# Sparse attention and two feed-forward stages: the values as the stationary operand, the probabilities divided by their sums on GpSimd

## The chip, the core and the metric

The program runs on one core of a Trainium2 chip. What is measured is the device time of one execution in microseconds, from the first to the last instruction. TensorE does the matmuls, VectorE the search and elementwise work, ScalarE activations and copies out of PSUM, GpSimd (POOL in the profile) elementwise work in SBUF; SyncE issues the transfers. The engines run side by side, each its own instructions in order, and wait for each other by semaphores.

## What is computed

Attention over 4 batches, 8 heads, 576 tokens and 64 dimensions a head, in which each query keeps its 32 best keys, and then two feed-forward stages over all 2304 tokens:

```python
scores = scale * np.matmul(q, k.transpose(0, 1, 3, 2))
kth = np.partition(scores, -top_k, axis=-1)[..., -top_k:-top_k + 1]   # top_k = 32
scores = np.where(scores >= kth, scores, -1000000000.0)
attn = np.exp(scores - np.max(scores, axis=-1, keepdims=True))
attn = attn / (np.sum(attn, axis=-1, keepdims=True) + 1e-09)
x = np.matmul(attn, v)                      # heads side by side: 2304 x 512
h = x @ w_in                                # 512 x 2048
x = (h / (1.0 + np.exp(-1.702 * h))) @ w_out
out = (((x @ w1) * (x @ w2)) @ w3) @ w_out2
```

## The kernel before

**Tiles and slots.** The 2304 tokens are eight chunks of 288 queries, two to a batch. A chunk has 18 tiles (`CT`), two groups of nine (`GT`), a group for four heads. Tile `r == 0` of a group is the left tile: the last 32 queries of each of the four heads, 128 rows. The others are 128 queries of one head; heads go in order, `j` being the half of the head's 256 queries. All tiles are in one sequence of 144, and a slot is one tile's turn. Each engine goes through the slots and in each does steps of several tiles, older ones further on: `slot.next(-3)` is the tile three behind.

**A tile's way.** TensorE makes scores two slots ahead (L560); ScalarE copies them to SBUF (L769, a ring of six rows). VectorE searches: four times the eight largest (L979, L987, L993, L999), three times replacing them (L984, L990, L996); the first half in the tile's own slot, the rest in the next. GpSimd scales the 32nd value to a threshold (`scale_threshold`, L1241) at the end of that next slot. In slot +2 ScalarE makes a penalty (L780), GpSimd subtracts it (L1227), ScalarE takes the exponential with its row sum (L789). In slot +3 GpSimd adds 1e-9 to the sum (`add_eps`, L1250), VectorE inverts it (`invert`, L1007), and TensorE transposes the row in five pieces (L573, L574). ScalarE copies them to `probs_T` (L798, L799) and TensorE multiplies, `probs_T` stationary and the values moving (L588): ten instructions in the profile for five matmuls. ScalarE copies the 64 columns out, scaled by the inverse sum (`copy_output`, L817; four pieces of all four heads' product for a left tile, L814). When both heads of a pair are there, TensorE transposes 128x128 of x in slot +4 (`transpose_x`, L603), and in slot +5 ScalarE makes its high half-precision part (`high_xt`, L831) and VectorE the low one (`low_xt`, L1028); for a left tile each in two instructions.

**Feed-forward.** The chunk before the current one, or the one before that, runs through the first feed-forward stage in the same slots: 32 units of twelve fp16 matmuls of 288 columns (L632), two in most slots, one in slots 3, 7, 12 and 16, the first from slot 5. Units 0 to 15 go through ScalarE (tanh L853, copy L856), VectorE (gate L1014), ScalarE (g_high L865) and GpSimd (g_low L1256).

**Preparation.** GpSimd splits the next group's queries into two parts (L1182): per group eight instructions of 256 columns and two of 128, and, when the next group belongs to a new batch, four of 576 for its keys. They lie in slots 1 to 5 of a group's nine. Keys come with even chunks, so the splits with keys stand in slots 1 to 5 of even chunks (for their second group) and in slots 10 to 14 of odd ones (for the first group of the next).

**Order on each engine, per slot.** It is written out by hand. TensorE: transpose_probs(-3), scores(+2), first unit, weigh_values(-3), second unit, transpose_x(-4). ScalarE: high_xt(-5), penalise(-2), second unit's copies, copy_probs(-3), copy_scores(+2), exponentials(-2), high gate, first unit's copies, copy_output(-3), preparation, high gate. VectorE: search of the new and the old tile in turn, gates between, invert(-3) and low_xt(-5) after the old tile's last replacement. GpSimd:

```python
add_eps(slot.next(-3))
subtract_penalty(slot.next(-2))
for c, u in second_unit(slot.next(-2)):
    low_gate(c, u)
negate_max(slot)
prepare(slot)
for c, u in first_unit(slot.next(-1)):
    low_gate(c, u)
scale_threshold(slot.next(-1))
```

**The end.** The second stage begins when all tiles and units are done, at some 975 us, and is matmuls alone.

## Time and profile before

| | us |
|---|---|
| three runs, median | 1276.18 |
| lowest, highest | 1272.49, 1278.28 |
| profiled execution, span | 1276.3 |
| busy: TensorE (weight loads) | 1179.1 (989.6) |
| busy: VectorE | 939.7 |
| busy: ScalarE | 788.3 |
| busy: GpSimd | 544.5 |

The profiled execution has no other time than its span; it equals the median. Busy times are unions: the instructions of one engine overlap at their ends. "L1028 waited for L831" means that the engine was idle before its instruction of line 1028 until one of line 831 released it.

### The profile page before, as it was taken

What the parts mean: (1) busy time and instruction counts of PE and PEld (TensorE: products, weight loads), DVE (VectorE), ACT (ScalarE), POOL (GpSimd) and SP (SyncE); (2) the same over time, 40 slices, a digit from 0 to 9 for tenths busy, and PEclk for the clock granted to TensorE, in tenths of its full rate; (3) what the DMA queues carried; (4) which work ended last, traced back from release to release, by engine and by line L of the source; (5) the groups of instructions that cost most, each with busy time, mean ns of one, the idle gap of its engine ahead of it and who ended that gap; (6) DMA issues with size and microseconds to landing.
All of it is one profiled execution on the core that took longest, in us unless ns stands there. A gap on an engine that the chain in (4) does not pass through costs nothing.

```text
span 1276.3 us, 25043 instructions
## 1 busy us (share of the span) xinstructions
PE 1179.1 (92%) x7798; PEld 989.6 (78%) x7798; DVE 939.7 (74%) x1974; ACT 788.3 (62%) x1806; POOL 544.5 (43%) x905
## 2 busy tenths in 40 slices
PE   2699987799999989999989999999989999999999
PEld 2466565687788877878868787887768999999998
DVE  4999999998999998999999899999442311302302
ACT  3655688867977977886886788797473222222211
POOL 4634445846755675674575666555230000000000
PEclk9799999899999989999999999999999999999999
DMA  9924142311001120000202100000151011011000
GB/s 283 361 60 158 58 128 86 99 35 48 2 26 45 42 65 29 25 11 24 62 22 62 44 11 25 11 7 1 37 206 44 9 41 49 8 41 49 0 25 25
DMA packets 29868, 75.40 MB, mean 59 GB/s; under 512 B 2480, under 2 KB 14256, under 8 KB 27824
## 3 DMA queue, kind: packets, MB, share of 16 engines
q1 hardware_dynamic: 29744, 73.93, 18.6%
q8 instruction: 55, 0.90, 0.3%
q14 instruction: 69, 0.57, 0.1%
HBM read 62.39 MB, written 11.53 MB: 58 GB/s over the span
## 4 chain that ended last, share of the span: by engine, by line
PE 56%; DVE 15%; issue 14%; ACT 6%; POOL 6%; DMA 1%; POOLq 0%; SPq 0%; ACTq 0%; DVEq 0%
PE ff_ps L632 32%; PE values_ps L588 9%; PE scores_ps L632 5%; PE scores_ps L560 4%; PE values_ps L632 3%; PE probs_T_ps L573 2%; DVE search L996 2%; DVE search L990 2%; POOL g_low L1256 2%; DVE top L987 2%; DVE peaks L1032 2%; DVE top L979 2%; DVE search L984 1%; ACT penalty L780 1%; ACT probs_T L798 1%
## 5 line engine op out<-in xcount | busy, mean ns | idle before, releaser
L1227 POOL TENSOR_TENSOR scores<-scores,penalty 128x576 f32<-128x576 f32 x144 | 203.2, 1411 | 196.2 <-ACT penalty L780 196.1
L588 PE MATMUL values_ps<-v_rows,probs_T 128*128 128x64 f32 (+3 forms) x1440 | 226.5, 295 | 53.9 <-ACT probs_T L799 46.3
L588 PEld LDWEIGHTS values_ps<-v_rows,probs_T 128*128 128x128 f32 (+1 forms) x1440 | 194.9, 193 | 100.9 <-ACT probs_T L799 66.0
L1160 DVE TENSOR_TENSOR ab_T<-a_sb,ff_ps 128x384 f32<-128x384 f32 x48 | 26.6, 554 | 211.1 <-PE ff_ps L632 211.1
L632 PE MATMUL ff_ps<-g_high,w_out_high 128*128 128x288 f16 x512 | 149.6, 292 | 2.7 <-DVE w_out_low L1019 1.6
L632 PE MATMUL ff_ps<-x_T_high,w_in_high 128*128 128x288 f16 x512 | 149.1, 291 | 2.9 <-ACT gate L856 2.8
L632 PE MATMUL ff_ps<-g_high,w_out_low 128*128 128x288 f16 x512 | 148.7, 291 | 0.0
L632 PE MATMUL ff_ps<-g_low,w_out_high 128*128 128x288 f16 x512 | 148.7, 290 | 0.0
L632 PE MATMUL ff_ps<-x_T_high,w_in_low 128*128 128x288 f16 x512 | 147.9, 289 | 0.0
L632 PE MATMUL ff_ps<-x_T_low,w_in_high 128*128 128x288 f16 x512 | 147.9, 289 | 0.0
L780 ACT ACTIVATE penalty<-scores,threshold_scaled 128x576 f32<-128x576 f32 x144 | 111.0, 771 | 35.6 <-POOL threshold_scaled L1241 35.1
L789 ACT ACTIVATE scores<-scores,neg_max 128x576 f32<-128x576 f32 x144 | 111.8, 776 | 32.1 <-POOL scores L1227 32.1
L1256 POOL TENSOR_TENSOR g_low<-gate,g_high 128x288 f16<-128x288 f32 x128 | 99.9, 782 | 72.4 <-ACT g_high L865 72.4
L632 PE MATMUL ff_ps<-x_high,w_high 128*128 128x384 f32 x384 | 128.4, 334 | 0.8 <-issue 0.8
L632 PE MATMUL ff_ps<-x_high,w_low 128*128 128x384 f32 x384 | 128.3, 334 | 0.0
L632 PE MATMUL ff_ps<-x_low,w_high 128*128 128x384 f32 x384 | 128.3, 334 | 0.0
L979 DVE MAX8 top<-scores 128x8 f32<-128x576 f32 x144 | 107.8, 749 | 5.8 <-ACT scores L769 3.7
L769 ACT ACTIVATE scores<-scores_ps 128x576 f32<-128x576 f32 x144 | 92.4, 641 | 27.0 <-PE scores_ps L560 26.9
L987 DVE MAX8 top<-search 128x8 f32<-128x576 f32 x144 | 107.5, 747 | 0.5
L999 DVE MAX8 top<-search 128x8 f32<-128x576 f32 x144 | 106.7, 741 | 0.0
L993 DVE MAX8 top<-search 128x8 f32<-128x576 f32 x144 | 106.6, 740 | 0.0
L990 DVE MATCH_REPLACE8 search<-top,search 128x576 f32<-128x576 f32 x144 | 106.6, 740 | 0.0
(116 smaller groups left out, 2777.1 us busy)
## 6 DMA issues: line engine op xcount, KB each, us to landing
q_stage<-q_T SPq DMA_DIRECT2D x32, 288.0 KB, 4.3
k_stage<-k_T SPq DMA_DIRECT2D x16, 576.0 KB, 8.4
x_scratch<-x_out SPq DMA_DIRECT2D x32, 144.0 KB, 1.7
x_T<-x_scratch SPq DMA_DIRECT2D x6, 768.0 KB, 4.8
out<-y_out SPq DMA_DIRECT2D x18, 256.0 KB, 2.0
v_rows<-v_rows_in SPq DMA_DIRECT2D x8, 512.0 KB, 3.6
w_T<-w_T_in SPq DMA_DIRECT2D x1, 4096.0 KB, 26.9
whole_weight<-w_in SPq DMA_DIRECT2D x2, 2048.0 KB, 11.1
```

What stands on the lines that cost most here:

```text
L588: last = nc.tensor.matmul(xp[:, 0:n], pt[0:rows, j * P:(j + 1) * P], vn[0:rows, j, first:first + n], start=j == 0, stop=j == KB)
L632: last = nc.tensor.matmul(out, stationary[i], moving[j], start=first and n == 0, stop=last_one and n == 2)
L769: act.activation(sc[:, t.ring(RING), :].rearrange("p (a b) -> p a b", a=2), ps[:, :, 0:HALF], ACT.Copy).then_inc(s_copied, 1)
L780: act.activation(pen[:, :], sc[:, t.ring(RING), :], ACT.Relu, bias=thr[:, r:r + 1], scale=-PENALTY).then_inc(pen_done, 1)
L789: act.activation(sc[:, t.ring(RING), :], sc[:, t.ring(RING), :], ACT.Exp, bias=negm[:, r:r + 1], scale=SCALE, accum_out=total[:, r:r + 1]) ...
L979: nc.vector.max(tops[:, 0:8], row).then_inc(search_a, 1)
L987: nc.vector.max(tops[:, 8:16], rest).then_inc(search_a, 1)
L990: nc.vector.match_replace(rest, tops[:, 8:16], rest, FLOOR).then_inc(search_a, 1)
L993: nc.vector.max(tops[:, 16:24], rest).then_inc(search_b, 1)
L999: nc.vector.max(tops[:, 24:32], rest).then_inc(search_b, 1)
L1227: pool.tensor_tensor(row, row, pen[:, :], ALU.subtract).then_inc(masked_done, 1)
L1256: pool.tensor_tensor(gt[1][:, u, :], gf[:, u % FF_RING, :], gt[0][:, u, :], ALU.subtract).then_inc(g_low, 1)
```

## The change

The values become the stationary operand (128 keys by one head's 64 dimensions) and the transposed probabilities move (128 queries). The product is then x already transposed, 64 rows by 128 queries, and two heads fill one PSUM tile, the even one in rows 0 to 63 and the odd one in rows 64 to 127. The order of tiles within a group becomes two heads in turn for one half of the queries, so that a pair is complete with every second tile (`ends_group`), and the matmuls of both tiles are issued together, alternating between the heads; a left tile makes its two pairs at once with 32 moving columns for each head. `transpose_x`, `copy_output`, `x_rows` and `x_left` go. Since rows of queries are now columns, the division by the row sum moves ahead of the transposes: `normalise` on GpSimd multiplies the 128x576 row by the inverse in place, in slot +3, and TensorE transposes, copies and weighs in slot +4. The last piece of the row is transposed as its last 128 columns, and `v_rows` holds zeros for the 64 keys that this counts twice. `probs_T` gets two rows, `x_T_ps` two banks; ScalarE copies all 640 columns in one instruction.

```diff
-        self.h, self.j = self.g * HG + (self.r - 1) // 2, (self.r - 1) % 2
+        self.h = self.g * HG + (self.r - 1) // 4 * 2 + (self.r - 1) % 2
+        self.j = (self.r - 1) // 2 % 2
...
+    def ends_group(self):
+        return self.r % 2 == 0
...
             def transpose_probs(t):
-                pe.wait_ge(exp_done, t.count(1))
+                pe.wait_ge(norm_done, t.count(1))
                 wait(pe, pt_copied, t.count())
                 row = sc[:, t.ring(RING), :]
-                for j in range(KB):
-                    nc.tensor.transpose(ptp[:, j * P:(j + 1) * P], row[:, j * P:(j + 1) * P], ident[:, :])
-                nc.tensor.transpose(pte[0:KR, 0:P], row[:, KB * P:S], ident[:, :]).then_inc(transposed, 1)
+                for j in range(KB + 1):
+                    last = nc.tensor.transpose(ptp[:, j * P:(j + 1) * P], row[:, min(j * P, S - P):min((j + 1) * P, S)],
+                                               ident[:, :])
+                last.then_inc(transposed, 1)

             def weigh_values(t):
-                pe.wait_ge(pt_copied, t.count(1))
-                wait(pe, o_copied, t.count())
-                first, n = (t.g * HG * D, HG * D) if t.left else (t.h * D, D)
-                for j in range(KB + 1):
-                    rows = KR if j == KB else P
-                    last = nc.tensor.matmul(xp[:, 0:n], pt[0:rows, j * P:(j + 1) * P],
-                                            vn[0:rows, j, first:first + n], start=j == 0, stop=j == KB)
+                wait(pe, xt_low, t.group_count(-2))
+                wait_alone(pe, pt_copied, t.count(1), passed_pe)
+                out = xq[t.group() % 2]
+                if t.left:
+                    members = [[(t, 2 * pair + odd, slice((2 * pair + odd) * LEFT, (2 * pair + odd + 1) * LEFT),
+                                 slice(pair * LEFT, (pair + 1) * LEFT)) for odd in range(2)] for pair in range(2)]
+                else:
+                    members = [[(t.next(odd - 1), t.next(odd - 1).h % HG, slice(0, P), slice(0, P))
+                                for odd in range(2)]]
+                for pair in members:
+                    for j in range(KB + 1):
+                        for odd, (tile, head, queries, cols) in enumerate(pair):
+                            first = (t.g * HG + head) * D
+                            last = nc.tensor.matmul(
+                                out[odd * D:(odd + 1) * D, cols], vn[:, j, first:first + D],
+                                pt[:, tile.ring(2), j * P + queries.start:j * P + queries.stop],
+                                start=j == 0, stop=j == KB)
                 last.then_inc(av_done, 1)
...
-                    transpose_probs(slot.next(-3))
+                    transpose_probs(slot.next(-4))
...
-                    weigh_values(slot.next(-3))
+                    weigh_values(slot.next(-4))
...
-                    transpose_x(slot.next(-4))
...
             def copy_probs(t):
-                wait(act, av_done, t.count())
-                act.activation(pt[:, 0:KB * P], ptp[:, :], ACT.Copy)
-                act.activation(pt[0:KR, KB * P:(KB + 1) * P], pte[0:KR, 0:P], ACT.Copy
-                               ).then_inc(pt_copied, 1)
+                wait(act, av_done, t.next(-2).group_count())
+                act.activation(pt[:, t.ring(2), :], ptp[:, 0:PADDED], ACT.Copy).then_inc(pt_copied, 1)
...
             def high_xt(t):
-                act.wait_ge(xt_made, t.xt_count(1))
+                act.wait_ge(av_done, t.group_count())
-                for rows, dst, src in xt_parts(t, xt[0]):
-                    last = act.activation(dst, src, ACT.Copy, scale=scale[rows, 0:1])
-                last.then_inc(xt_high, 1)
+                act.activation(xt_place(t, xt[0]), xt_source(t), ACT.Copy, scale=scale[:, 0:1]).then_inc(xt_high, 1)
...
-                    copy_probs(slot.next(-3))
+                    copy_probs(slot.next(-4))
...
-                    copy_output(slot.next(-3))
...
             def low_xt(t):
-                for (rows, dst, src), (_, high, _) in zip(xt_parts(t, xt[1]), xt_parts(t, xt[0])):
-                    last = nc.vector.scalar_tensor_tensor(dst, src, scale[rows, 0:1], high, ALU.mult, ALU.subtract)
-                last.then_inc(xt_low, 1)
+                nc.vector.scalar_tensor_tensor(xt_place(t, xt[1]), xt_source(t), scale[:, 0:1], xt_place(t, xt[0]),
+                                               ALU.mult, ALU.subtract).then_inc(xt_low, 1)
...
+            def normalise(t):
+                wait_alone(pool, recip_done, t.count(1), passed_pool)
+                r = t.ring(4)
+                row = sc[:, t.ring(RING), :]
+                pool.tensor_scalar(row, row, rinv[:, r:r + 1], 1.0, ALU.mult, ALU.mult).then_inc(norm_done, 1)
...
                     for c, u in first_unit(slot.next(-1)):
                         low_gate(c, u)
+                    normalise(slot.next(-3))
                     scale_threshold(slot.next(-1))

-            pool.memset(xl[:, :, :], 0.0).then_inc(ones_set, 1)
+            pool.memset(vn[0:P - KR, KB, :], 0.0).then_inc(zeros_set, 1)
```

## Rows read from the trace of the kernel before

**Rows 1.** Table of stretches: us; busy (instructions) PE, PEld, DVE, ACT, POOL; clock, DMA, GB/s.

```profile
600.00:700.00 100.00, 91.91 (x693) 76.77 (x692) 91.98 (x208) 78.58 (x192) 62.34 (x102) 0.98 0.19 48
1000.00:1100.00 100.00, 100.00 (x534) 94.30 (x533) 20.35 (x35) 22.65 (x40) 0.00 (x0) 1.00 0.09 32
```

**Rows 2.** Waits, 300 to 900 us: who waited for whom, us in total, times, longest.

```profile
POOL scores L1227 <- ACT penalty L780: 140.9, 102, 2.9
...
ACT x_T_high L831 <- PE x_T_ps L603: 22.1, 22, 2.3
...
DVE x_T_low L1028 <- ACT x_T_high L831: 14.9, 17, 1.6
...
DVE inverse_total L1007 <- POOL total_eps L1250: 5.5, 7, 1.1
```

**Rows 3.** The gate on DVE: groups of 300 to 900 and 885 to 1000 us, one instruction.

```profile
L1014 DVE SCALAR_TENSOR_TENSOR gate<-tanh,gate 128x288 f32<-128x288 f32 x96 | 57.9, 603 | 2.1 <-ACT gate L856 2.1
...
L1014 DVE SCALAR_TENSOR_TENSOR gate<-tanh,gate 128x288 f32<-128x288 f32 x17 | 7.3, 453 | 9.4 <-ACT gate L856 9.4
...
658.64 1.16 DVE L1014 SCALAR_TENSOR_TENSOR gate<-tanh,gate 128x288 f32<-128x288 f32 x1
```

**Rows 4.** Table of stretches again: chunks 4 and 5, slots 1-5, 10-14, then slot 17.

```profile
487.70:517.90 30.20, 28.69 (x209) 23.74 (x208) 25.96 (x60) 23.78 (x52) 19.60 (x32) 0.94 0.11 34
541.50:572.20 30.70, 27.66 (x205) 22.19 (x204) 30.43 (x70) 28.19 (x74) 23.46 (x40) 1.00 0.01 2
592.50:620.40 27.90, 27.54 (x211) 22.82 (x210) 25.79 (x61) 21.53 (x50) 15.59 (x30) 1.00 0.05 17
645.60:679.20 33.60, 27.58 (x205) 22.14 (x203) 31.68 (x69) 30.21 (x74) 28.05 (x42) 1.00 0.06 19
...
680.00:700.00 20.00, 20.00 (x152) 17.44 (x151) 18.33 (x43) 11.69 (x27) 8.47 (x18) 0.93 0.41 98
```

**Rows 5.** DVE's waits in 487 to 512, 592 to 615 and 645 to 680 us.

```profile
DVE inverse_total L1007 <- POOL total_eps L1250: 1.4, 2, 0.9
...
DVE x_T_low L1028 <- ACT x_T_high L831: 2.1, 2, 1.1
...
DVE inverse_total L1007 <- POOL total_eps L1250: 1.1, 1, 1.1
```

**Rows 6.** Groups by line on POOL, whole span, shapes apart.

```profile
L1227 POOL TENSOR_TENSOR scores<-scores,penalty 128x576 f32<-128x576 f32 x144 | 203.2, 1411 | 196.2 <-ACT penalty L780 196.1
...
L1182 POOL TENSOR_TENSOR q_high_low<-q_stage,q_high_low 128x256 fp32r<-128x256 f32 x64 | 45.6, 732 | 4.0 <-ACT q_high_low L745 4.0
...
L1273 POOL MEMSET q_left_high_low<- 128x1280 f32 x1 | 1.2, 1164 | 0.0
```

**Rows 7.** Timeline of POOL from a threshold on: start, us, instruction.

```profile
572.81 0.21 POOL L1241 TENSOR_SCALAR threshold_scaled<-top 128x1 f32<-128x1 f32 x1
...
573.91 1.42 POOL L1227 TENSOR_TENSOR scores<-scores,penalty 128x576 f32<-128x576 f32 x1 [0.60 <-ACT penalty L780]
```

**Rows 8.** Timeline of DVE from a last maximum to the next reciprocal.

```profile
580.55 0.74 DVE L999 MAX8 top<-search 128x8 f32<-128x576 f32 x1
...
584.70 0.15 DVE L1007 RECIPROCAL inverse_total<-total_eps 128x1 f32<-128x1 f32 x1
```

**Rows 9.** Timelines of PE cut inside a run, for spacings: values, transposes.

```profile
575.80 1.36 PE L588 MATMUL values_ps<-v_rows,probs_T 128*128 128x64 f32 x10
...
576.73 0.43 PE L588 MATMUL values_ps<-v_rows,probs_T 64*128 64x64 f32 x2
...
573.23 0.60 PE L573 MATMUL probs_T_ps<-identity,scores 128*128 128x128 f32 x4
...
573.45 0.38 PE L573 MATMUL probs_T_ps<-identity,scores 128*128 128x128 f32 x2
```

**Rows 10.** Groups by line on ACT, 300 to 900 us.

```profile
L817 ACT ACTIVATE x_rows<-values_ps,inverse_total 128x64 f32<-128x64 f32 x92 | 28.7, 312 | 20.1 <-PE values_ps L588 19.5 <-issue 0.3
L799 ACT ACTIVATE probs_T<-probs_T_end_ps 64x128 f32<-64x128 f32 x103 | 27.1, 264 | 0.0
```

## What the change should do to the time

> **What bounds the kernel now.** I read the table of stretches first. In steady attention both VectorE and TensorE are busy 92% of the 100 us shown, ScalarE 79%, GpSimd 62%; from 1000 us on TensorE alone is busy, at 100% [rows 1]. The change touches nothing in that last part, so it can only act on the attention part, 144 tiles of 5.83 us each (600 us by 103 tiles).
>
> TensorE's busy share misleads. Its matmuls overlap; what counts is their spacing: the first of ten value instructions starts at 575.80, the ninth at 576.73, so they stand 0.116 us apart [rows 9]. Counted so, a slot (one tile's turn) asks 24 feed-forward matmuls at 0.123, four score matmuls at 0.13, five transposes at 0.11 and the values at 1.16 (some 2.2 for a left tile, whose ten have 256 columns, twice a transpose's), some 5.2 us. VectorE has its search whatever happens: seven instructions of 0.74 [rows 8], which overlap by a little and so stand some 0.66 apart, and three value loads of 0.07: 4.8 us, some 4.9 with the reciprocal, and about 1 more in a slot with two gates. VectorE is the bound, and the gain is in its idle time. Two waits make nearly all of it: on x_T_high 14.9 us and on total_eps 5.5 us, of 600 [rows 2].
>
> Where they lie is seen in four stretches of five slots each [rows 4]: slots 1 to 5 of an even chunk (VectorE idle 30.20 - 25.96 = 4.2 us), slots 10 to 14 of an even one (0.3), slots 1 to 5 of an odd one (2.1), slots 10 to 14 of an odd one (1.9), and 1.7 around slot 17 of an odd one. In the first and the last of these POOL splits new keys as well as queries, and VectorE waits for total_eps; in the odd slots 1 to 5 it waits for x_T_high alone [rows 5].
>
> **Part 1: one instruction more on GpSimd.** `normalise` is a TENSOR_SCALAR over 128x576 fp32, 144 times. The trace of before has no such instruction. From below: the one-element form costs 0.21 us [rows 7], and a memset, which only writes, 0.91 ns an element (1164 ns for 1280), so 0.21 + 0.52 = 0.73 us. From above: the two-input subtraction of the same shape, 1.41 us, 2.13 ns an element (1.411 less 0.732, by 320 elements) [rows 6]. Between them: if its pace is set by the inputs read, one instead of two halves the slope, 0.21 + 576 x 1.07 ns = 0.83 us; if the write's 0.91 and the reads add up, 0.21 + 576 x (0.91 + 0.61) = 1.09. I take 0.84 and call it n: the memset's write is cheaper than one of the two reads would be, and can lie beside it.
>
> The Trainium skill (GPSIMD Engine Reference, section 3.1 on the element loop) gives 1.8 cycles an element as the best case of a tight loop and 2.6 for two inputs; the second agrees with the 2.13 ns above. By the first n would be an estimated 1.08 us, and the sum below 1269.
>
> Its place matters more than its price: `normalise(slot-3)` stands before `scale_threshold(slot-1)`, and behind that stands `add_eps`, which releases VectorE's `invert`, an instruction in the middle of its search. POOL's own loop is: threshold, ScalarE's penalty, subtraction, negated maximum, preparation, gates, threshold. From the end of the threshold to the start of the subtraction it takes at least 573.91 - 573.02 = 0.89 us, add_eps within [rows 7]. A slot without preparation or gates so costs 0.89 + 1.41 + 0.21 + 0.21 = 2.7 us, each gate 0.74, and nine tiles' preparation 8 x 0.73 + 2 x 0.5 = 6.8 us, with keys 4 x 1.41 more, 12.5. How late may POOL be? The last maximum ends at 581.29 and the reciprocal after it starts at 584.70; less the threshold and add_eps themselves (0.7) that leaves 2.7 us [rows 8]; in slots with two gates about 1 to 1.3 us more, so 4.
>
> Now the stretches, with n = 0.84:
> - Even, 1 to 5: POOL asks 13.6 + 12.5 + 4.2 = 30.3 against VectorE's 26.0. With 0.6 brought in and 2.7 to spare VectorE stalls 2.2 us, where it stalls 4.2 now. Three chunks: gain 6.0.
> - Odd, 1 to 5: 13.6 + 6.8 + 4.2 = 24.6 against 25.8. POOL keeps up, and the waits for x_T_high go (part 2). Three times 2.1: gain 6.3.
> - Even, 10 to 14, nine gates (6.7): 13.6 + 6.8 + 6.7 + 4.2 = 31.3 against 30.4; covered by the 4 us to spare, even with 1.5 brought in (an estimate; ScalarE, busy 28 of 31 us there now, brings in the lag and gets lighter).
> - Odd, 10 to 14: 13.6 + 12.5 + 7.0 + 4.2 = 37.3 against 31.7; 5.6 + 1.5 - 4 = 3.1 stalled, now 1.9. Two chunks: loss 2.4.
> - Slot 17: gain 1.6.
> Sum: 11.5 us. It moves by 2.5 us for each 0.1 us of n: 14 at 0.73, 6 at 1.07; at 1.41 it is -3, and -7 with the even slots 10 to 14 stalling too.
>
> A second price of POOL being busier: VectorE's gate has two SBUF inputs and takes 0.603 us beside a working POOL but 0.453 after the search, where POOL mostly idles [rows 3]. 0.15 us for a busy share of 0.63 is 0.24; n adds a share of 0.14, so 0.034 us on 112 gates, 3.9 us. Bounds: 0, if a one-input instruction doesn't disturb it, and 8, if it hits gates as the key splits do (one gate there takes 1.16 [rows 3]).
>
> **Part 2: x arrives transposed.** Gone are ten transposes of x per chunk, `copy_output` (16 copies of 0.312, and 4 of 0.306 for each of two left tiles) and the second copy of probs_T (0.264); the first grows from 512 to 640 columns, by some 0.1 [rows 10]. ScalarE loses about 0.5 us a slot and, more to the point, no longer waits at the head of its slot for a transpose that TensorE issued last in its own: 22.1 us of waits [rows 2], behind which stand the penalty and POOL's subtraction, which waited 140.9 us. high_xt now waits for values issued before TensorE's second unit of the slot before. What is late next is POOL, as counted. The left tiles' low_xt becomes one instruction instead of two (0.28 us spaced); 14 of 16 lie where VectorE bounds: 4.0 us.
>
> **Part 3: the values matmul.** Before, weights of 128 columns paced each 64-column matmul at 0.116, 2.3 us for two tiles. After, a pair has 20 instructions of 128 moving columns, and by the transposes' spacing (two from 573.23 to 573.45) each takes 0.11 [rows 9]. If the two heads, in different columns of the array, run at once, a pair costs some 1.1 us; if not, 2.2. Left tiles: 40 instructions of 32 columns; from 1.1 us (pairs at once) to 4.4 (0.11 each), now 2.2. All of this is beside VectorE's work except in the last five slots, after the search, where TensorE has the feed-forward left: 5 x 0.6 = 3 us if at once, 0 if not; I take 2. The pair falls in every second slot, so TensorE's slots alternate by about 1 us either side; scores are made two slots ahead, which covers it.
>
> The Trainium skill (TensorEngine Tiling (Array Packing), Key Properties) says that changing the tiling mode drains the array. No run here shows it yet. It would speak against the change 20 times a chunk, and would be a rival below.
>
> `transpose_probs` moves to slot-4 and waits for norm_done; behind it on TensorE are the scores and both units. normalise is done one slot earlier, so at POOL's largest allowed lag TensorE waits about 1 us, which VectorE doesn't see. Five buffers and counters (two probs_T rows, two x_T banks, the memset of 64 rows of v_rows for that of x_left) I cost at nothing: the rows are freed a slot ahead, and the memset is some 0.3 us more in a start that waits for the first loads.
>
> **Sum.** 1276.3 (the profiled span, equal to the median of 1276.18) - 11.5 - 4.0 + 3.9 - 2 = 1263, 1% less.
>
> **Rivals.**
> - A: the halves don't run at once, and each change of shape costs. TensorE then asks 47 (384 feed-forward matmuls) + 12.5 (96 for scores) + 9.9 (90 transposes) + 17.6 (eight pairs) + 2 x 3.3 (left tiles, between the bounds) = 94 us a chunk, as before, plus 20 changes of an estimated 0.15 (a little over one spacing), 97 of 105. For it: transposes and values alternate in each slot. Against: VectorE still asks more over a chunk. In light slots (4.88 us) TensorE at 5.3 becomes the bound for some seven of 18: 0.4 x 7 x 7 chunks less what VectorE would stall anyway, about 10 us given back: 1272.
> - B: n is 1.41 or more. POOL's loop with the keys then bounds: -7 - 8 + 4 = 11 us lost: 1287. It turns slower from n of about 1.35, or lower if gates suffer fully. For it: every full-width POOL instruction in the trace costs that; the added one sits in the loop. Against: all of those read two inputs.
> - C: n is about 1.07: 1269.
> - D: POOL's lag is absorbed better than counted (less brought in, cheap n): up to 25.7 us of idle and 4 of low_xt could go, less some 5 us of stalls: 1252.
>
> **How the numbers follow.** Forecast (n of 0.75 to 0.95, halves at once) 0.42; A 0.18; B 0.15; C 0.13; D 0.12. The range takes in D and the lower half of B: 1249 to 1283. This kernel's measurement tells about 0.5% (6.4 us) from no change, so faster is under 1269.8 and slower over 1282.6. Faster: nearly all of the forecast and D, half of C, a fifth of A: 0.60. Slower: most of B and a little of A: 0.17. Same: 0.23.
>
> **What would show it.** TENSOR_SCALAR scores near 0.84 us; VectorE's waits for x_T_high nearly gone and those for total_eps larger, in slots 1 to 5 of even and 10 to 14 of odd chunks; value matmuls of two heads starting together; gates a few hundredths longer. It is wrong if POOL waits for the reciprocal ahead of normalise for long (then the chain through invert is a loop that I have not counted), or if TensorE, waiting for norm_done, lets the scores run late and VectorE waits for them.

## The result and the profile after

| | before | after |
|---|---|---|
| median of six runs, us | 1275.87 | 1282.55 |
| lowest, highest | 1272.49, 1278.28 | 1280.74, 1287.76 |
| span of the profiled execution | 1276.3 | 1280.7 |
| end of the last maximum of the last search | 905.8 | 910.2 |

The kernel became slower: the ratio is 1.0062, with an interval of 1.004 to 1.0084. 1263 was forecast; 1282.55 lies at the very edge of the range that was given (1249 to 1283), on the wrong side of no change. From the last maximum to the end both kernels take 370.5 us, so the 4.4 us between the two spans arise while VectorE searches. (After the change a run is timed 1.8 us above its span. The span of before is therefore rather that of one of its longer runs, not of its median, and that makes up the 2.3 us between 4.4 and the 6.7 of the medians. What follows compares span with span.)

The busy times of the changed kernel are these: engine, busy us, share, instructions.

```profile
PE 1090.9 (85%) x8198; PEld 889.5 (69%) x8198; DVE 941.8 (74%) x1958; ACT 731.4 (57%) x1454; POOL 670.0 (52%) x1049
```

TensorE lost 88 us of work and ScalarE 57; GpSimd got 126 more. VectorE, the bound, has as much as before. Engines off the bound got lighter, and the time went up.

The table of stretches of the changed kernel, same slots and columns as [rows 4] (slot 17 left out):

```profile
489.90:517.90 28.00, 23.75 (x227) 19.12 (x226) 25.65 (x60) 19.97 (x37) 22.48 (x35) 0.94 0.10 34
542.70:575.00 32.30, 25.39 (x235) 19.50 (x234) 30.20 (x68) 26.11 (x62) 27.92 (x43) 0.95 0.01 2
595.00:620.40 25.40, 23.87 (x240) 19.27 (x239) 25.40 (x60) 19.38 (x37) 20.07 (x35) 1.00 0.05 19
648.40:681.80 33.40, 23.04 (x219) 18.12 (x217) 32.84 (x69) 25.67 (x56) 29.81 (x42) 0.95 0.06 19
```

Slots 1 to 5 are 2.2 and 2.5 us shorter, as hoped. Slots 10 to 14, the ones with gates, are 1.6 longer in the even chunk and 0.2 shorter in the odd one, although there VectorE's idle time fell from 1.9 to 0.6: its busy time rose by 1.2, with as many instructions (69).

VectorE's waits until its last maximum, before and then after (who waited for whom: us in total, times, longest):

```profile
DVE x_T_low L1028 <- ACT x_T_high L831: 17.3, 19, 1.6
DVE inverse_total L1007 <- POOL total_eps L1250: 6.8, 9, 1.1
DVE gate L1014 <- ACT gate L856: 2.1, 8, 0.4
```

```profile
DVE inverse_total L980 <- POOL total_eps L1222: 16.8, 24, 1.3
...
DVE x_T_low L1000 <- ACT x_T_high L807: 7.0, 3, 6.3
DVE gate L987 <- ACT gate L831: 5.5, 11, 1.0
```

The 19 waits for x are three, and one of these alone is 6.3 us long: it is another thing, below. The waits for `total_eps`, that is for GpSimd, went from 6.8 to 16.8. The groups of `gate` and of `low_xt` for full tiles on VectorE in the same stretch (count, busy us, mean ns, idle before), before and after:

```profile
L1014 DVE SCALAR_TENSOR_TENSOR gate<-tanh,gate 128x288 f32<-128x288 f32 x112 | 70.9, 633 | 2.1 <-ACT gate L856 2.1
L1028 DVE SCALAR_TENSOR_TENSOR x_T_low<-x_T_ps,scale,x_T_high 128x128 f16<-128x128 f32 x62 | 21.1, 341 | 15.9 <-ACT x_T_high L831 15.0
```

```profile
L987 DVE SCALAR_TENSOR_TENSOR gate<-tanh,gate 128x288 f32<-128x288 f32 x112 | 81.9, 731 | 5.9 <-ACT gate L831 5.5
L1000 DVE SCALAR_TENSOR_TENSOR x_T_low<-x_T_ps,scale,x_T_high 128x128 f16<-128x128 f32 x61 | 20.2, 331 | 7.0 <-ACT x_T_high L807 7.0
```

The 112 gates grew by 11.0 us. And the new instruction on GpSimd, over the whole span:

```profile
L1230 POOL TENSOR_SCALAR scores<-scores,inverse_total 128x576 f32<-128x576 f32 x144 | 122.5, 851 | 12.4 <-DVE inverse_total L980 12.4
```

**The long wait.** In chunk 1, between 225 and 275 us, the chain is seen in the waits of the changed kernel, first SyncE's, then ScalarE's and VectorE's; the last row is SyncE's wait for the same buffer before the change:

```profile
SPq L393 <- PE x_T_ps L599: 17.8, 1, 17.8
```

```profile
ACT w_out_high L850 <- DMA piece<-w_out: 7.3, 1, 7.3
...
DVE x_T_low L1000 <- ACT x_T_high L807: 6.3, 1, 6.3
```

```profile
SPq L391 <- PE values_ps L588: 5.3, 1, 5.3
```

SyncE's list has `load_v`, which overwrites the values of the batch before, ahead of three pieces of the weights. It waits for the last values matmul of the old group. That matmul moved one slot back, and in that slot TensorE first stood 5.5 us for `normalise` (until 227.12): it began at 232.24, where before it began at 223.29. So the list stood for 17.8 us instead of 5.3, and the pieces behind it were issued late:

```profile
233.75 0.37 SPq L393 DMA_DIRECT2D v_rows<-v_rows_in  x1
234.16 0.52 SPq L396 DMA_DIRECT2D v_rows<-v_rows_in  x1
234.72 10.63 SPq L440 DMA_DIRECT2D piece<-w_out  x3
```

(SyncE's timeline after: start, us, instruction.) Before, the pieces began at 226.98. ScalarE waited 7.3 us for a piece, with `high_xt` behind that in its order, and VectorE waited 6.3 for `high_xt`.

### The profile page after: what moved, and what is told of

It reads as the page before. It is cut to its first block, busy times and chain, and to the rows that moved or that the text cites. A ratio compares the mean times of both kernels' runs of the same rounds, so it can differ in the third digit from the quotient of the medians.

```text
span 1280.7 us, 25399 instructions
## 1 busy us (share of the span) xinstructions
PE 1090.9 (85%) x8198; PEld 889.5 (69%) x8198; DVE 941.8 (74%) x1958; ACT 731.4 (57%) x1454; POOL 670.0 (52%) x1049
## 4 chain that ended last, share of the span: by engine, by line
PE 36%; DVE 22%; issue 20%; POOL 17%; ACT 3%; DMA 1%; POOLq 1%; DVEq 1%; SPq 0%; ACTq 0%
PE ff_ps L630 23%; PE scores_ps L630 5%; DVE search L963 4%; POOL scores L1230 4%; POOL g_low L1236 3%; DVE search L969 3%; DVE top L960 3%; POOL scores L1199 3%; DVE top L952 3%; PE x_T_ps L630 3%; DVE search L957 2%; DVE peaks L1004 2%; PE scores_ps L562 2%; PE probs_T_ps L575 2%; PE x_T_ps L599 2%
## 5 line engine op out<-in xcount | busy, mean ns | idle before, releaser
L575 PE MATMUL probs_T_ps<-identity,scores 128*128 128x128 f32 x720 | 115.1, 294 | 148.8 <-POOL scores L1230 145.3
L575 PEld LDWEIGHTS probs_T_ps<-identity,scores 128*128 128x128 f32 x720 | 84.5, 148 | 185.9 <-POOL scores L1230 178.4
L630 PE MATMUL ff_ps<-x_T_high,w_in_high 128*128 128x288 f16 x512 | 154.0, 301 | 2.8 <-ACT gate L831 2.8
L630 PE MATMUL ff_ps<-x_T_low,w_in_high 128*128 128x288 f16 x512 | 152.8, 298 | 0.0
L630 PE MATMUL ff_ps<-x_T_high,w_in_low 128*128 128x288 f16 x512 | 152.5, 298 | 0.0
L1230 POOL TENSOR_SCALAR scores<-scores,inverse_total 128x576 f32<-128x576 f32 x144 | 122.5, 851 | 12.4 <-DVE inverse_total L980 12.4
L599 PEld LDWEIGHTS x_T_ps<-probs_T,v_rows 128*64 128x64 f32 x1920 | 92.9, 143 | 34.1 <-issue 34.1
L599 PE MATMUL x_T_ps<-probs_T,v_rows 128*64 128x128 f32 (+1 forms) x1920 | 110.0, 266 | 7.6 <-ACT probs_T L796 6.5
L796 ACT ACTIVATE probs_T<-probs_T_ps 128x640 f32<-128x640 f32 x144 | 100.5, 698 | 16.0 <-PE probs_T_ps L575 15.4
L960 DVE MAX8 top<-search 128x8 f32<-128x576 f32 x144 | 107.5, 746 | 0.7 <-issue 0.2
```

Source lines behind the costliest of these rows:

```text
L575: last = nc.tensor.transpose(ptp[:, j * P:(j + 1) * P], row[:, min(j * P, S - P):min((j + 1) * P, S)], ident[:, :])
L599: last = nc.tensor.matmul(out[odd * D:(odd + 1) * D, cols], vn[:, j, first:first + D], pt[:, tile.ring(2), j * P + queries.start:j * P + q ...
L630: last = nc.tensor.matmul(out, stationary[i], moving[j], start=first and n == 0, stop=last_one and n == 2)
L796: act.activation(pt[:, t.ring(2), :], ptp[:, 0:PADDED], ACT.Copy).then_inc(pt_copied, 1)
L960: nc.vector.max(tops[:, 8:16], rest).then_inc(search_a, 1)
L1230: pool.tensor_scalar(row, row, rinv[:, r:r + 1], 1.0, ALU.mult, ALU.mult).then_inc(norm_done, 1)
```

## The experiments

Every time is a median with its ratio to the kernel before on the same chip; differences in us are against 1282.55, the changed kernel, of which each is a variant where nothing else is said. The experiments ran on several chips; the kernel before has medians of 1274.9 to 1276.5 on them, so a difference of a us or two between two variants says little.

### e1_v_load_last: is the queue's stall worth its 6.3 us

```diff
                     load_piece(12)
-                    load_v(chunk, 0)
                     for i in range(13, 2 * PIECES):
                         load_piece(i)
+                    load_v(chunk, 0)
```

> The changed kernel, with one line of SyncE's list moved: in chunk 2 the load of v_rows for the first group stands behind the last three weight pieces and not ahead of them. In the changed kernel SyncE stood 17.8 us on that load (it waits for the values matmuls of the group that last read v_rows, which now end a slot later and group by group), ScalarE waited 7.3 us for a w_out piece and VectorE 6.3 us behind it, once, at 233 us; before the same wait of SyncE was 5.3 us and VectorE had none. Theory Q (a transfer queued behind a moved wait): the 6.3 us idle goes, 1282.5 becomes 1276 to 1278. Rival: the piece would have been late anyway, because it also waits for VectorE's low part of the piece before; then under 1.5 us is gained.

Measured: 1275.76, ratio 0.9997 (0.998 to 1.0015), 6.8 us less. SyncE's wait at the values' load is no longer among its waits of that stretch, and VectorE's for `x_T_high` are gone until 905 us; the waits for `total_eps` stay:

```profile
DVE inverse_total L980 <- POOL total_eps L1222: 16.9, 24, 1.3
...
DVE gate L987 <- ACT gate L831: 6.7, 12, 1.1
```

So two swapped lines on an engine that computes nothing are worth all that the change lost. They turn it into no change, and no more: the 13 us of gain that were forecast are still missing.

### e2_threshold_first: does normalise hurt by standing ahead of the threshold

```diff
-                    normalise(slot.next(-3))
                     scale_threshold(slot.next(-1))
+                    normalise(slot.next(-3))
```

> The changed kernel, with GpSimd's normalise(slot-3) behind scale_threshold(slot-1) and not ahead of it, nothing else. Theory L (normalise costs because it stands in the loop threshold, penalty, subtraction, threshold): the 0.85 us then lie in the gap in which GpSimd waits for ScalarE's penalty, at least 0.89 us long; VectorE's waits for total_eps fall from 16.8 us to under 9 and the time by 6 to 10 us, to 1273 to 1277. Rival G (the cost is GpSimd's being busy, which slows VectorE's two-input gate, 0.611 us a gate before and 0.696 now over 128 gates, 10.9 us): the gates stay at 0.69 and the time stays within 3 us of 1282.5.

Measured: 1278.62, 1.0028 (1.0008 to 1.0048), 3.9 us less. VectorE's waits until 905 us:

```profile
DVE gate L987 <- ACT gate L831: 10.0, 12, 1.4
DVE inverse_total L980 <- POOL total_eps L1222: 9.4, 16, 1.0
```

The expectation (1273 to 1277) was missed. Waiting for `total_eps` fell by 7.4, but the gates' wait for ScalarE rose by 4.5. (The profiled run is 3.4 us above the median, so its waits show where time goes, but they can't be added up to the 3.9.) The reason is one step further on: `norm_done` comes later, TensorE's transposes with it, and ScalarE, which copies them, waited in 300 to 900 us for them 38.1 us where it had waited 6.1. Whichever of the two goes first, the other's chain is late.

### e3_one_column: what normalise costs altogether

```diff
-                act.activation(pt[:, t.ring(2), :], ptp[:, 0:PADDED], ACT.Copy)
+                act.activation(pt[:, t.ring(2), :], ptp[:, 0:PADDED], ACT.Copy, scale=2.0 ** -6)
...
-                pool.tensor_scalar(row, row, rinv[:, r:r + 1], 1.0, ALU.mult, ALU.mult)
+                pool.tensor_scalar(row[:, 0:1], row[:, 0:1], rinv[:, r:r + 1], 1.0, ALU.mult, ALU.mult)
```

> The changed kernel, whose normalise works on one column of the row instead of 576; the division of the other columns is left out, and the copy of probs_T scales by a constant so that x stays in range. All waits and the order stay. It prices the width of normalise alone (0.85 to about 0.22 us a tile). Theory L and G together: waits for total_eps back to about 7 us, gates back to 0.61, 1282.5 becomes 1262 to 1267. If the cost of the change lies elsewhere (the longer way of a tile, TensorE's alternate slots), it stays above 1275. The stall of SyncE's list (6.3 us) may stay in either case.

The kernel leaves out the division of 575 of the 576 columns, so it is a price and not a version. Measured: 1256.35, 0.9842 (0.9818 to 0.9866), 26.2 us less, more than the 16 to 20 expected, with the stall of SyncE's list still in it (5.9 of VectorE's waits). Waiting for `total_eps` fell to 4.7:

```profile
DVE inverse_total L980 <- POOL total_eps L1222: 4.7, 9, 0.8
```

The gates came down only to 682 ns (76.4 us) and their waits to 1.5. These are 12.1, 5.5 and 4.0 us; 1.1 is a shorter stall. Some 3.5 of the 26.2 I did not follow. The rest of the change, transposed x without the full-width division on GpSimd, is thus worth about 20 us against the kernel before: the idea was good, and its price sits in one instruction.

### e4_on_scalar: the division on ScalarE, where copy_output had stood

```diff
+            def normalise(t):
+                act.wait_ge(recip_done, t.count(1))
+                r = t.ring(4)
+                row = sc[:, t.ring(RING), :]
+                act.activation(row, row, ACT.Copy, scale=rinv[:, r:r + 1]).then_inc(norm_done, 1)
...
+                    normalise(slot.next(-3))
                     prepare(slot)
```

> The changed kernel with normalise on ScalarE, an ACTIVATE Copy scaled by the inverse sum over the same 128x576, where copy_output stood before; GpSimd does none of it. Theories L and G: GpSimd is as light as before the change, ScalarE gets 144 x 0.65 to 0.78 us and stays under 90% busy; waits for total_eps about 7 us, gates 0.61 us, 1264 to 1269. Rival S (ScalarE becomes the late engine in the slots with gates and preparation, where it was busy 28 of 31 us before): VectorE waits for total_eps or for ScalarE's gate copies by over 15 us and the time is 1278 or more.

(`normalise` is taken off GpSimd's list.) Measured: 1253.01, 0.9818 (0.9795 to 0.9841), 29.5 us less, where 14 to 19 were expected. On ScalarE the instruction takes 778 ns. VectorE's waits and its gates until 879 us:

```profile
DVE x_T_low L1009 <- ACT x_T_high L815: 2.3, 2, 2.0
DVE inverse_total L989 <- POOL total_eps L1231: 1.4, 3, 0.6
```

```profile
L996 DVE SCALAR_TENSOR_TENSOR gate<-tanh,gate 128x288 f32<-128x288 f32 x112 | 82.0, 732 | 0.2
```

The waits are gone, but the gates are exactly as long as with `normalise` on GpSimd, which was busy 537 us here until 883, as against 655 until 910. So the gates do not pay for GpSimd's busy share. That reading of mine falls here.

What they pay for is seen when each gate is sorted by what GpSimd did meanwhile (my count from the timelines, of all 128 gates without the first 16; the last 16, after the search, are in the first row; at least 0.1 us in common; count and mean us; left out are cases with splits, and ten after the change with both `normalise` and g_low, of 0.77):

| GpSimd beside the gate | before | after | on ScalarE |
|---|---|---|---|
| nothing of size | 63: 0.44 | 32: 0.44 | 52: 0.44 |
| g_low alone | 28: 0.65 | 2: 0.68 | 19: 0.65 |
| normalise alone | | 11: 0.49 | |
| the subtraction, with or without g_low | 7: 0.78 to 1.01 | 42: 0.89 to 0.92 | 30: 1.07 to 1.12 |

Most of the cost is in meeting the subtraction of the penalty, the longest of GpSimd's instructions. One such meeting, DVE's and POOL's timelines of the changed kernel:

```profile
621.48 1.58 DVE L987 SCALAR_TENSOR_TENSOR gate<-tanh,gate 128x288 f32<-128x288 f32 x1
```

```profile
621.33 1.42 POOL L1199 TENSOR_TENSOR scores<-scores,penalty 128x576 f32<-128x576 f32 x1 [0.60 <-ACT penalty L777]
```

The gate begins 0.15 us behind the subtraction and ends 0.31 behind it: it takes 1.58 where it takes 0.44 alone. This is no slowing in proportion but a hold. Of the 112 gates of full tiles until the last maximum, 55 before the change and 76 after it last longer than 0.46 us, and every one of them began while a GpSimd instruction was under way and ended 0.30 to 0.32 us behind that instruction's end; the others all take 0.43 to 0.46 (three of them, which met only the last 0.13 us of a subtraction, are counted below too). So a gate's price is what is left of GpSimd's instruction when the gate begins. Counted by what held them (gates, us over 0.44 each):

| held by | before | after | on ScalarE |
|---|---|---|---|
| the subtraction | 16: 9.6 | 48: 23.4 | 36: 24.8 |
| g_low | 26: 5.8 | 11: 4.2 | 17: 3.9 |
| a split | 13: 6.3 | 17: 4.2 | 12: 4.2 |
| normalise | | 3: 0.9 | |

The difference, 11.0 us, is the growth of the gates. `normalise`, which has one input, holds them too, if a gate begins well inside it; a gate that begins just behind its start goes first, and `normalise` takes 1.05 us instead of 0.75. Of the first kind is the gate at 759.39, of the second the one at 740.50:

```profile
759.39 0.74 DVE L987 SCALAR_TENSOR_TENSOR gate<-tanh,gate 128x288 f32<-128x288 f32 x1
...
740.50 0.44 DVE L987 SCALAR_TENSOR_TENSOR gate<-tanh,gate 128x288 f32<-128x288 f32 x1
```

```profile
759.08 0.75 POOL L1230 TENSOR_SCALAR scores<-scores,inverse_total 128x576 f32<-128x576 f32 x1
...
740.41 1.05 POOL L1230 TENSOR_SCALAR scores<-scores,inverse_total 128x576 f32<-128x576 f32 x1
```

The three gates that it held began 0.26 to 0.38 us into it and took 0.68 to 0.78; in e9 it held seven, of 0.51 to 0.86. Five gates began 0.08 to 0.09 us behind its start and went first, as did four that began within 0.03 us of the start of a g_low or a split (three before, one after). The mean of 0.49 in the first table is that low because only two of its eleven gates were held. Here a page of the Trainium skill bears: GPSIMD Engine Reference (Specifications) says that GpSimd shares its SBUF interfaces with VectorE, and that they contend when VectorE's instruction has two SBUF inputs, as the gate has. The trace agrees, for GpSimd's instructions with two inputs and with one, and adds the price: the rest of that instruction and 0.31 us.

### e5_scalar_v_last: both repairs

```diff
-                    load_v(chunk, 0)
                     for i in range(13, 2 * PIECES):
                         load_piece(i)
+                    load_v(chunk, 0)
...
+                    normalise(slot.next(-3))
                     prepare(slot)
```

> normalise on ScalarE (as in e4_on_scalar) and the load of v_rows behind the last weight pieces (as in e1_v_load_last), to see whether the two add up and how far the version goes. In e4 VectorE still waited 2.0 us in chunk 1 behind that piece, where the changed kernel waited 6.3. Theory Q: 1.5 to 2.5 us under e4, 1251; if the two do not add, it stays at 1253.

Measured: 1249.23, 0.9791 (0.9768 to 0.9815), 3.8 us below the one before. Of VectorE's waits behind chunk 0 only one for `total_eps` of 0.6 us is left, and gates of 726 ns. The stall was smaller with ScalarE's order (2.0), so the list gives less here than the 6.8 of e1: the two repairs don't add up in full. (1.5 to 2.5 us were expected.)

### e6_transposes_late: would later transposes relieve the loop

```diff
-                    transpose_probs(slot.next(-4))
                     scores(slot.next(2))
                     for c, u in first_unit(slot):
                         unit(c, u)
+                    transpose_probs(slot.next(-4))
...
-                    weigh_values(slot.next(-4))
                     for c, u in second_unit(slot):
                         unit(c, u)
+                    weigh_values(slot.next(-4))
```

> The changed kernel with two steps moved in TensorE's slot: transpose_probs(slot-4) stands behind scores and the first unit, weigh_values(slot-4) behind the second unit. TensorE stood 87 us (300 to 900 us) at the head of its slot on normalise, with scores and both units behind it. Theory E (this wait is one of the costs, through feed-forward blocks, their gate copies and VectorE's gates that come late, 5.9 us of waits for the gate copy against 2.1 before): the waits for the gate copy fall under 2 us and the time by 3 to 6 us, to 1277 to 1279. Rival: VectorE and GpSimd alone set the pace and the wait is idle time; then within 2 us of 1282.5, or slower, since high_xt then waits for values that end a slot's second unit.

Measured: 1313.97, 1.0294 (1.0255 to 1.0332), 31.4 us more: wrong in sign. VectorE's waits until 920 us:

```profile
DVE inverse_total L980 <- POOL total_eps L1222: 41.8, 42, 1.8
DVE x_T_low L1000 <- ACT x_T_high L807: 20.4, 8, 4.0
```

TensorE's 87 us of waits at the head of its slot for `normalise` looked like a cost in the changed kernel; this run can't price them by themselves, since it moves the values too. Ending the slot with the values instead puts x late for ScalarE, whose `high_xt` opens its slot, and the penalty, the subtraction and `add_eps` are late behind it. Of the two orders the one with the long wait on TensorE is the cheap one.

### e7_gate_later: take the first gate out of the subtraction's way

```diff
                     search(old, 4)
-                    for c, u in first_unit(old):
-                        gate(c, u)
                     search(new, 1)
                     search(old, 5)
                     invert(slot.next(-3))
+                    for c, u in first_unit(old):
+                        gate(c, u)
```

> The changed kernel with VectorE's first gate moved from behind search(old, 4) to behind invert, some 1.5 us later in the slot. Theory H (a gate takes 0.44 us beside an idle GpSimd and 0.9 to 1.5 beside its two-input subtraction; in the changed kernel GpSimd is on time in odd chunks and its subtraction falls on the first gate, 42 of 112 gates against 7 before, while beside normalise alone a gate takes 0.49): the first gates fall between the subtraction's end (2.5 us into the slot) and, in even chunks, its start (3.5 to 5); mean gate from 0.70 to 0.50 to 0.58 us, 12 to 20 us less work on VectorE, of which 6 to 12 us show: 1271 to 1277. Rival G (the gates are slow because GpSimd is busier in all, so anywhere): mean gate stays at 0.66 or more and the time within 3 us.

Measured: 1263.93, 0.9909 (0.9884 to 0.9933), 18.6 us less, with the division still on GpSimd. Until 890 us:

```profile
L987 DVE SCALAR_TENSOR_TENSOR gate<-tanh,gate 128x288 f32<-128x288 f32 x112 | 62.8, 561 | 0.0
```

```profile
DVE inverse_total L980 <- POOL total_eps L1222: 27.1, 27, 2.1
...
DVE x_T_low L1000 <- ACT x_T_high L807: 3.3, 1, 3.3
```

The gain is larger than the 6 to 12 us expected. The gates lose 19.1 us and their waits 5.5; the stall of the list is halved (3.0), and 10.3 comes back as waiting for `total_eps`, since `invert` now comes earlier in VectorE's slot than GpSimd can serve it. 17.3 of the 18.6 are so accounted for. The held gates show it: the subtraction holds 15 here, for 2.6 us over 0.44 in all, where it held 48 for 23.4.

### e12_before_gate_later: the same move in the kernel before

```diff
                     search(old, 4)
-                    for c, u in first_unit(old):
-                        gate(c, u)
...
                     invert(slot.next(-3))
+                    for c, u in first_unit(old):
+                        gate(c, u)
```

> The kernel before the change with its first gate behind invert. There GpSimd is late in most slots and the subtraction (3.5 to 5 us into the slot) misses the first gate, which takes 0.44 us in 63 of 112 cases. Theory H: little to win in the gates (78 us, at most 6 us less), and in odd chunks, slots 6 to 10, the subtraction ends at 3.4 and meets the moved gate: 1272 to 1280. If the move gains 8 us or more here too, the gain in e7 is not the collision that the change brought but something of the order itself.

Measured: 1268.16, 0.9931 (0.9899 to 0.9963), 7.7 us below the kernel before (8.0 below its median on the same chip), and so at the very bound of 8 that would have spoken for "something of the order itself". The gates did not shorten there, and the waits for x fell, until 899 us:

```profile
L1014 DVE SCALAR_TENSOR_TENSOR gate<-tanh,gate 128x288 f32<-128x288 f32 x112 | 72.5, 647 | 0.0
```

```profile
DVE x_T_low L1028 <- ACT x_T_high L831: 13.0, 15, 1.7
```

So the move is good by itself, by covering other waits: 2.1 of the gates' own and 4.3 of those for x; the rest of the 7.7 I did not follow (the profiled run is the slowest of the five). Only the rest of e7's gain, some 11 of 18.6, belongs to what the change had brought. The gate's length is the part that exists only after the change (70.9 to 72.5 here, 81.9 to 62.8 there).

### e8_heads_in_turn: is it the alternation that makes the heads concurrent

```diff
-                    for j in range(KB + 1):
-                        for odd, (tile, head, queries, cols) in enumerate(pair):
+                    for odd, (tile, head, queries, cols) in enumerate(pair):
+                        for j in range(KB + 1):
```

> The changed kernel whose two heads of a pair are not alternated: five matmuls of the one, then five of the other. It shows what the alternation gives TensorE. In the changed kernel two matmuls of different heads start 6 ns apart and the next pair 109 ns later, 1.1 us for 20. If only neighbours in different columns overlap: 20 x 0.109 = 2.2 us for a pair. The time: within 3 us of the changed kernel if TensorE is not the bound; 5 us or more over it if it is.

One run alone: 1294.88, 12.3 us more, and 7 above the longest of the changed kernel's six. A pair in TensorE's timeline with its neighbours, at full clock in both, first the changed kernel's, then this one's:

```profile
589.07 0.29 PE L630 MATMUL ff_ps<-g_high,w_out_low 128*128 128x288 f16 x1
589.29 1.31 PE L599 MATMUL x_T_ps<-probs_T,v_rows 128*64 128x128 f32 x20
590.53 0.30 PE L630 MATMUL ff_ps<-g_high,w_out_high 128*128 128x288 f16 x1
```

```profile
588.73 2.02 PE L599 MATMUL x_T_ps<-probs_T,v_rows 128*64 128x128 f32 x20
590.68 0.30 PE L630 MATMUL ff_ps<-g_high,w_out_high 128*128 128x288 f16 x1
```

Twenty instructions take 1.24 us to the next matmul if the heads alternate, 1.95 if not. That 0.7 of a pair should matter on an engine that waits 87 us for transposes is seen in ScalarE's waits until 905 us, after and here:

```profile
ACT x_T_high L807 <- PE x_T_ps L599: 28.0, 30, 3.1
```

```profile
ACT x_T_high L807 <- PE x_T_ps L599: 48.8, 39, 3.4
```

The values end TensorE's first half of a slot, and `high_xt`, at the head of ScalarE's, waits for them; `total_eps` is then waited for 28.9 us instead of 16.8. The Trainium skill (TensorEngine Tiling (Array Packing), Key Properties) says that tiles operate independently, which these rows show, and that a change of tiling mode drains TensorE. A change is in the rows above: the first value matmul starts 0.22 us behind the feed-forward one where those stand 0.12 apart, and where this step took 0.12 too before the change (medians of 79 and 64 such steps). A tenth of a us, 20 times a chunk, is 2 of TensorE's 105 us; it decides nothing.

### e9_penalty_first: take the penalty out from behind high_xt

```diff
-                    high_xt(slot.next(-5))
                     penalise(slot.next(-2))
+                    high_xt(slot.next(-5))
```

> The changed kernel with one step moved on ScalarE: penalise(slot-2) ahead of high_xt(slot-5), not behind it. ScalarE still stood 22.0 us (300 to 900 us) at the head of its slot on values, with the penalty and so GpSimd's subtraction behind it; before it was 22.1 us on the transpose of x. Theory X (this wait did not go, it only changed its releaser, and it is what keeps GpSimd late): VectorE's waits for total_eps fall from 16.8 us to under 11 and the time by 4 to 8 us, to 1275 to 1279. Rival: GpSimd is late by its own work (normalise in its loop) and the waits for total_eps stay within 2 us of 16.8; VectorE then waits for x_T_high instead and nothing is gained.

Measured: 1280.19, 1.0042 (1.0018 to 1.0065), 2.4 us less. Until 905 us:

```profile
DVE x_T_low L1000 <- ACT x_T_high L807: 15.7, 20, 6.3
...
DVE inverse_total L980 <- POOL total_eps L1222: 6.9, 11, 1.1
```

9.9 us of waiting for `total_eps` are gone and 8.7 for x are back, the wait that the change was to remove. The link (`high_xt` late, so the penalty, so the subtraction, so `add_eps`) is shown; the 4 to 8 us expected did not come, since ScalarE can't serve both first.

### e13_gate_later_v_last: how much the list still gives with the gate moved

```diff
-                    load_v(chunk, 0)
                     for i in range(13, 2 * PIECES):
                         load_piece(i)
+                    load_v(chunk, 0)
...
                     search(old, 4)
-                    for c, u in first_unit(old):
-                        gate(c, u)
...
                     invert(slot.next(-3))
+                    for c, u in first_unit(old):
+                        gate(c, u)
```

> The changed kernel, normalise left on GpSimd, with both small moves: v_rows loaded behind the last weight pieces (e1: 6.8 us) and the first gate behind invert (e7: 18.6 us). If the two are separate costs they add: 1282.5 - 6.8 - 18.6 = 1257, and what then stays against e10_scalar_gate_later (1242.9) is the price of normalise on GpSimd, 14 us, seen as waits for total_eps of over 20 us. If e7 had already taken the queue's stall away (its VectorE waited 3.3 us for it in chunk 1 and not 6.3), only 2 to 4 us come on top: 1260 to 1262.

Measured: 1260.64, 0.9879 (0.9845 to 0.9914): 3.3 us less than e7, not 6.8. That is what VectorE still waited at the stall in e7, though the intervals of the two ratios overlap. One wait of size is left:

```profile
DVE inverse_total L980 <- POOL total_eps L1222: 26.1, 27, 2.1
```

### e10_scalar_gate_later: all three repairs

```diff
-                    load_v(chunk, 0)
                     for i in range(13, 2 * PIECES):
                         load_piece(i)
+                    load_v(chunk, 0)
...
+                    normalise(slot.next(-3))
                     prepare(slot)
...
                     search(old, 4)
-                    for c, u in first_unit(old):
-                        gate(c, u)
...
                     invert(slot.next(-3))
+                    for c, u in first_unit(old):
+                        gate(c, u)
```

> e5_scalar_v_last (normalise on ScalarE, v_rows loaded behind the pieces: 1249.2) with the first gate behind invert, as in e7_gate_later. e5 has no wait of VectorE left but 5.8 us for its first scores and one for the instruction stream; its gates take 88.5 us where 128 x 0.44 = 56 would do. Theory H: gates fall to under 70 us, and since nothing else is late most of it shows: 1232 to 1240. Rival: as GpSimd follows a faster VectorE, the subtraction moves onto the gate again, and the time stays over 1245.

Measured: 1242.92, 0.9743 (0.9716 to 0.9769), 39.6 us below the changed kernel and the best of all, if short of the 1232 to 1240 expected. Until 870 us:

```profile
DVE inverse_total L989 <- POOL total_eps L1231: 3.0, 9, 0.5
```

Its gates are at 637 ns, those of before. From e13 it differs only in the engine of the division: 17.7 us. Waiting for `total_eps` falls by 23.1 (26.1 to 3.0), and the gates grow by 8.1 (63.2 to 71.3), since with an earlier GpSimd the subtraction holds 26 of them again (15.3 us); that is 15.0 of the 17.7.

## Why the prediction was wrong, point by point

Three steps failed: SyncE's list was costed at nothing and cost 6.3 us; the gates were to pay 3.9 us by a busy share and paid 11.0 by coincidence; and 17.5 us of VectorE's waits were left where 12.6 were forecast, because ScalarE's wait at the head of its slot did not go. Against the kernel before, span with span (until the last maximum, us):

| term | forecast | measured |
|---|---|---|
| VectorE's waits for x and `total_eps`, without the stall | -11.5 | -6.6 (24.1 to 17.5) |
| gates longer | +3.9 | +11.0 |
| `low_xt` | -4.0 | some -6 |
| SyncE's list | nothing | +6.3 |
| gates waiting for ScalarE's copy | nothing | +3.4 |
| last five slots and the end | -2 | 0 |
| small things (reciprocal, `w_out_low`) | nothing | some -3.5 |
| sum | -13.6 | +4.6; the spans say +4.4 |

The `low_xt` and small terms are worked out from the part of these instructions that overlaps no other one of VectorE, summed over the timelines; `low_xt` has 8.7 us less of it, of which 3.0 come back in the search instructions beside it.

**What held.** The size of Part 1's instruction: n was taken as 0.84 and is 0.851 in the mean, so B and C are out as sizes. That it fits so well is luck: where `normalise` meets neither a gate nor another of VectorE's instructions with two tensor inputs (101 of 144 times), it takes 0.75, near the lower bound of 0.73, and only what VectorE does to the other 43 lifts the mean. That the heads run at once; a left tile's forty instructions too take 1.29 us (568.43 to 569.72), near the lower end of 1.1 to 4.4. That VectorE's waits for x go: 17.3 us to 0.7 without the stall. That slots 1 to 5 gain: VectorE's idle time is 2.4 and 0.0 where 2.2 and 0 were forecast. That waiting for `total_eps` would grow.

**The step "I cost at nothing" in Part 3.** It looked at whether buffers are freed early enough, not at who waits for the freeing. `transpose_probs` and `weigh_values` were moved a slot, and with them `av_done`, for which SyncE's list waits ahead of each load of values, once with three pieces of weights behind it. Nothing in the text goes through SyncE's list. e1 shows its price, 6.8 us, half of the forecast's gain.

**The second price of Part 1, the gates.** +3.9 against +11.0, beyond the upper bound of 8 that was given. The row [rows 3] was right (0.603 and 0.453) and its reading wrong: a rate was made of it, 0.24 us for a full busy share. e4 refutes the rate: GpSimd's share falls and the gates stay at 732 ns. What counts is which instruction is under way when the gate begins, and how much of it is left. The lower bound, "if a one-input instruction doesn't disturb it", has a wrong reason as well: `normalise` holds a gate like the others, and costs only 0.9 us because just three gates began far enough inside it. The cost comes from the subtraction (9.6 to 23.4 us), which the change doesn't touch but shifts by a us or two, onto the first gate. In slots 6 to 12 of chunks 3 and 5 it begins 0.6 to 1.9 us into VectorE's slot after the change, 1.9 to 4.3 before, and the first gate stands at 1.3. That it is early because ScalarE's slot became lighter is argued, from e4 (GpSimd earlier still, meetings of 1.07 to 1.12 us) and e8 (GpSimd later, gates of 615 ns), and not shown by itself.

**The step "ScalarE no longer waits at the head of its slot".** [rows 2] had 22.1 us. The changed kernel, waits in 300 to 900 us:

```profile
POOL scores L1199 <- ACT penalty L777: 79.6, 101, 2.2
...
ACT x_T_high L807 <- PE x_T_ps L599: 22.0, 25, 2.2
...
DVE x_T_low L1000 <- ACT x_T_high L807: 0.7, 2, 0.4
```

The wait is as long as before. It had another releaser: pairs come in every second slot, and TensorE, waiting for `normalise` at the head of its slot, brings them late. The text saw TensorE's wait of about 1 us and said that VectorE doesn't see it; through `high_xt`, the penalty, the subtraction and `add_eps` VectorE does, as e6, e8 and e9 show. So GpSimd began each loop later than counted. In even slots 10 to 14, where 4 us to spare were to cover all, VectorE is idle 2.1 us ([rows 4]: 0.3), and in odd ones 0.6 where 3.1 were forecast: the loop was summed well, but what it brings in and what is to spare were not. Over all, 17.5 us of waits stand where 12.6 were forecast.

**The end.** No run followed the 2 us that the last slots were to give; both kernels take 370.5 us from the last maximum. This stays open, as do 3.5 us of e3's 26.2.

**The rivals.** None was the one. The case on the slower side, B, rested on n; the loss came by two ways at once that no rival had, a list that stood and a coincidence of two instructions. The upper end of the range, 1283, was there for B alone; that the measured time falls inside it is luck. TensorE's mean granted clock until the last maximum is 0.96 after and 0.97 before; no run prices this by itself.

## What to carry to other kernels

When a step moves, follow each of its semaphores to every engine that waits for it, the list of transfers first: one wait that ends later holds back everything queued behind it, and here that was worth more than the change's whole effect. When a VectorE instruction with two inputs in SBUF begins while GpSimd is at work, it ends only after GpSimd's instruction, so look where in the slot each lies before and after, and not at busy shares. A division that must go somewhere belongs on the engine that the same change has just relieved (here ScalarE), not on one that stands in the loop through VectorE's search.

## What the runs showed of the hardware

- Two column tiles of the array run at once: two fp32 matmul instructions of 128 columns in different halves start 7 ns apart and the next two 0.11 us after them, as one alone does in e8; that is 1.24 us for twenty with the step to the next matmul, and 1.95 if one half is issued after the other.
- Going from feed-forward matmuls to values matmuls in half the columns took 0.22 us, where full-width ones took 0.12.
- A gate with two SBUF inputs (128x288) takes 0.44 us alone. If it begins inside an instruction of GpSimd that has over 0.13 us left, it ends 0.31 us behind that instruction: 0.44 to 1.59 us with the subtraction of 576 columns, 0.68 to 0.78 with the one-input `normalise`. A gate that begins 0.08 to 0.09 us behind the start of `normalise` goes first in the changed kernel, and `normalise` takes 1.05 us.
- GpSimd's TENSOR_SCALAR of 128x576 fp32 takes 0.75 us where VectorE doesn't hold it, about half of the two-input form (1.41); with one column it is 0.27 (e3).
